# Two MLPs behind an attention, one core: another order on ScalarE and VectorE in the second unit of the second layer's later pairs

## The reference

```python
x = attn_out.reshape(B * S, D)                       # 6016 x 256
# first MLP
h = x @ w_in;  g = h * (1.0 / (1.0 + np.exp(-1.702 * h)));  x = g @ w_out
# second MLP
h = x @ w_in
g = np.where(h > 0.0, h, alpha * (np.exp(np.minimum(h, 0.0)) - 1.0))   # alpha = 1
return (g @ w_out).astype(np.float32)
```

## Time and profile before

| | us |
|---|---|
| median of 3 runs | 1035.35 |
| lowest and highest run | 1034.66, 1036.51 |
| the profiled execution, its own time | 1033.88 |
| its span in the profile | 1032.1 |
| PE busy in the span | 1023.7 |
| DVE busy | 762.9 |
| ACT busy | 760.8 |

### The profile page before, as it was taken

How to read it: one execution, slowest core, us unless ns; L and a number is a source line. 1 busy time by engine, 2 the same in 40 slices (tenths; PEclk the granted TensorE clock), 3 DMA queues, 4 the chain that set the end, 5 groups by cost and what they waited for, 6 DMA issues and landing times.

```text
span 1032.1 us, 14040 instructions
## 1 busy us (share of the span) xinstructions
PE 1023.7 (99%) x4636; PEld 860.1 (83%) x4636; DVE 762.9 (74%) x1244; ACT 760.8 (74%) x1362; POOL 26.1 (3%) x27
## 2 busy tenths in 40 slices
PE   8999999999999999999999999999999999999998
PEld 7878888888888888889998888888888888888996
DVE  6797766656656565655888988888888788788776
ACT  6996765565666566556688888788788788788885
POOL 3700000000000000000000000000000000000000
PEclk9999999999999999999999999999999999999999
DMA  8912012003003002003112002102102001110111
GB/s 328 325 38 55 1 41 42 0 21 62 1 1 80 1 1 59 1 1 122 42 61 98 1 1 62 21 1 62 21 1 62 15 6 38 20 21 1 21 22 36
DMA packets 103192, 46.25 MB, mean 45 GB/s; under 512 B 87184, under 2 KB 93776, under 8 KB 102480
## 3 DMA queue, kind: packets, MB, share of 16 engines
q1 hardware_dynamic: 102208, 44.12, 15.6%
q10 hardware_dynamic: 912, 1.25, 0.3%
HBM read 33.03 MB, written 12.32 MB: 44 GB/s over the span
## 4 chain that ended last, share of the span: by engine, by line
PE 98%; DMA 1%; ACT 0%; DVE 0%; SPq 0%; POOL 0%; issue 0%; ACTq 0%; DVEq 0%
PE bank L1155 32%; PE bank L1156 31%; PE bank L1157 31%; PE bank L1165 2%; DMA qk<-in_k_dram 1%; PE bank L1262 0%; PE bank L1263 0%; PE bank L1267 0%; SPq L337 0%; POOL qk_lo L441 0%; PE bank L1407 0%; ACT stage L470 0%; PE bank L1240 0%; PE bank L1178 0%; PE bank L1227 0%
## 5 line engine op out<-in xcount | busy, mean ns | idle before, releaser
L1155 PE MATMUL bank<-g_hi,w_dn_hi 128*128 128x512 f32 (+1 forms) x768 | 296.0, 385 | 0.0
L1156 PE MATMUL bank<-g_lo,w_dn_hi 128*128 128x512 f32 (+1 forms) x768 | 295.8, 385 | 0.0
L1157 PE MATMUL bank<-g_hi,w_dn_lo 128*128 128x512 f32 (+1 forms) x768 | 295.7, 385 | 0.0
L934 DVE TENSOR_TENSOR g_lo<-gated,g_hi 128x512 fp32r<-128x512 f32 (+1 forms) x384 | 259.8, 677 | 44.8 <-ACT g_hi L631 38.7
L1155 PE MATMUL bank<-blk_hi,w_up_hi 128*128 128x512 f32 (+1 forms) x672 | 260.2, 387 | 0.1
L1156 PE MATMUL bank<-blk_lo,w_up_hi 128*128 128x512 f32 (+1 forms) x672 | 258.9, 385 | 0.0
L1157 PE MATMUL bank<-blk_hi,w_up_lo 128*128 128x512 f32 (+1 forms) x672 | 258.8, 385 | 0.0
L631 ACT CAST g_hi<-gated 128x512 fp32r<-128x512 f32 (+1 forms) x288 | 175.8, 611 | 21.4 <-DVE gated L921 21.4
L1155 PEld LDWEIGHTS bank<-g_hi,w_dn_hi 128*128 128x128 f32 x768 | 144.2, 188 | 27.5 <-DVE g_lo L934 0.6
L1157 PEld LDWEIGHTS bank<-g_hi,w_dn_lo 128*128 128x128 f32 x768 | 144.2, 188 | 27.0
L1156 PEld LDWEIGHTS bank<-g_lo,w_dn_hi 128*128 128x128 f32 x768 | 144.2, 188 | 26.8
(11 more groups left out here) (125 smaller groups left out, 756.1 us busy)
## 6 DMA issues: line engine op xcount, KB each, us to landing
x_scratch<-xo SPq DMA_DIRECT2D x10, 512.0 KB, 3.1
raw<-x_scratch SPq DMA_DIRECT2D x5, 1024.0 KB, 4.9
out_dram<-blocks SPq DMA_DIRECT2D x40, 128.0 KB, 2.7
qk<-in_q_dram SPq DMA_DIRECT2D x13, 384.0 KB, 8.0
qk<-in_k_dram SPq DMA_DIRECT2D x12, 384.0 KB, 9.6
stage<-in_moe_w_in_dram SPq DMA_DIRECT2D x8, 512.0 KB, 7.7
stage<-in_moe_w_out_dram SPq DMA_DIRECT2D x8, 512.0 KB, 4.8
blocks<-in_v_dram SPq DMA_DIRECT2D x32, 128.0 KB, 3.3
```

What stands on the lines that cost most here:

```text
L934: nc.vector.tensor_tensor(g[1][:, x, 0:w], gated[:, n % 2, 0:w], g[0][:, x, 0:w].bitcast(F32), ALU.subtract).then_inc(c_glo, 1)
L1155: nc.tensor.matmul(out_ps, w_hi, x_hi, start=start, stop=False, skip_group_check=goes_on)
L1156: nc.tensor.matmul(out_ps, w_hi, x_lo, start=False, stop=False, skip_group_check=goes_on)
L1157: return nc.tensor.matmul(out_ps, w_lo, x_hi, start=False, stop=stop, skip_group_check=goes_on)
```

## The change

For the units with s > 6 and u = 1 (U = 57, 65, 73, 81, 89) ACT and DVE get an order of their own. ACT: copy_u1(U), Relu and Exp (U-1, H12), evacuate(s-1, 1), copy_u2(U), g_hi (U-1, H21), Relu and Exp (U, H11), copy_u3(U), g_hi (U, H11), and from there as before. DVE: sum12_of(U-1), elu (U-1, H21), g_lo (U-1, H22), sum11_of(U), elu (U-1, H12), g_hi (U-1, H12), g_lo (U-1, H21), g_lo (U-1, H12), elu (U, H11), g_lo (U, H11), sum22_of(U), elu (U, H22). All other units, and PE's, SP's and POOL's lists, stay as they are. No instruction is added or dropped.

```diff
@@ scalar, unit(U) @@
-                if u == 1 and s >= 1:
+                if u == 1 and s > NP:
+                    nonlinear(U - 1, H12)
                     evacuate(s - 1, 1)
-                if U - 1 < LAYER:
+                    copy_u2(U)
                     g_hi(U - 1, H21)
-                    gelu(U - 1, H12)
+                    nonlinear(U, H11)
+                    copy_u3(U)
+                    g_hi(U, H11)
                 else:
...
@@ vector, unit(U) @@
-                g_lo(U - 1, H21)
-                if U > LAYER:
+                if U // UNITS > NP and U % UNITS == 1:
                     elu(U - 1, H12)
-                g_hi(U - 1, H12)
-                if LAYER < U < ALL:
+                    g_hi(U - 1, H12)
+                    g_lo(U - 1, H21)
+                    g_lo(U - 1, H12)
                     elu(U, H11)
-                g_lo(U - 1, H12)
+                else:
...
```

More of the change, by code:

```diff
@@ L758, in unit @@
                     copy_u1(U)
-                if u == 1 and s >= 1:
+                if u == 1 and s > NP:
+                    nonlinear(U - 1, H12)
                     evacuate(s - 1, 1)
-                if U - 1 < LAYER:
+                    copy_u2(U)
                     g_hi(U - 1, H21)
-                    gelu(U - 1, H12)
-                else:
[L765 to L777, removed]
+                    nonlinear(U, H11)
+                    copy_u3(U)
+                    g_hi(U, H11)
+                else:
+                    if u == 1 and s >= 1:
+                        evacuate(s - 1, 1)
+                    if U - 1 < LAYER:
+                        g_hi(U - 1, H21)
+                        gelu(U - 1, H12)
+                    else:
+                        elu_first(U - 1, H12)
+                        g_hi(U - 1, H21)
+                        elu_second(U - 1, H12)
+                    if U == ALL:
+                        return
+                    nonlinear(U, H11)
+                    copy_u2(U)
+                    g_hi(U, H11)
+                    if u == 0:
+                        block_hi(s, T4)
+                    if U == LAYER - 1:
+                        dn_hi(2 * FB - 2)
+                    copy_u3(U)
                 side(U)
@@ L1119, in unit @@
                     sum11_of(U)
-                g_lo(U - 1, H21)
-                if U > LAYER:
+                if U // UNITS > NP and U % UNITS == 1:
                     elu(U - 1, H12)
-                g_hi(U - 1, H12)
-                if LAYER < U < ALL:
+                    g_hi(U - 1, H12)
+                    g_lo(U - 1, H21)
+                    g_lo(U - 1, H12)
                     elu(U, H11)
-                g_lo(U - 1, H12)
+                else:
+                    g_lo(U - 1, H21)
+                    if U > LAYER:
+                        elu(U - 1, H12)
+                    g_hi(U - 1, H12)
+                    if LAYER < U < ALL:
+                        elu(U, H11)
+                    g_lo(U - 1, H12)
                 if U == ALL:
```

## The result

| | changed | before, same comparison | ratio, 95% interval |
|---|---|---|---|
| first comparison, 9 and 9 runs | 1032.74 us | 1034.66 us | 0.998 (0.9972 to 0.9988) |
| second, 11 and 32 runs | 1033.68 us | 1034.0 us | 0.9996 (0.9987 to 1.0005) |
| third, 11 and 33 runs | 1033.53 us | 1034.82 us | 0.9982 (0.9973 to 0.9991) |

In the first comparison, the one that the prediction was about, the changed kernel is 1.9 us faster, 0.20%, and the interval doesn't hold 1. The forecast was 1033.7 us, 0.16% faster, with "no difference" as the likeliest verdict. The profiled execution took 1032.74 us, its span is 1031.0.

A forecast was written before the change was run, and what follows sets the result against it. TensorE, busy 99% of the span, was taken to bound the kernel. 1.8 us removed less about 0.15 given back took the profiled 1033.88 to 1032.2; the median's 1.5 above that gave 1033.7 us, range 1032.6 to 1035.2.

The forecast's parts named there:

- What bounds, and the prize: TensorE, busy 99%; its starts lost to late product5 and product7 loads in five units: 4 x 0.34 + 0.44 = 1.8 us.
- Part 1: ACT's Relu and Exp of (U-1, H12) ahead of the evacuation: product5's load no longer waits, 0.8 us to spare.
- Part 2: Evacuation behind that Exp: down H22's load 0.03 us late, last pair 0.13; costs 0 to 0.1, last 0.03 to 0.15.
- Part 3: copy u2 behind the evacuation, at product6's end: product7's load gets 1 us of room, down H21's 0.4 us.
- rival (c): product5 and product7 freed, but g_lo of H21 late for down H21: 1035.2 us; chance 0.09.
- Part 4: copy u3 ahead of g_hi (U, H11) delays sum22; next unit starts 0.55 us late on ACT, costing 0 to 0.1 per pair.
- Rival (a): Later sum22 makes next unit's copy u2 0.2 to 0.3 us late, product7 waits: 1034.3 us; chance 0.18.
- The price of lateness: At TensorE's weight loads, each may be about 0.1 us late at no cost; lateness beyond that is lost.
- The rule set beside the trace: Skill's 215.7 ns per 512-column matmul, against the trace's 0.2267 us: prize would be 2.1 us; the sum used the trace.
- net of 1.65 us: Whole kernel: 1.8 us removed, about 0.15 given back at the evacuation and in the next unit.
- the level: Median before, 1035.35 us, taken 1.5 above the profiled execution; the same difference added to 1032.2 gives 1033.7.
- (d): Matmul step really shorter, or lost starts pull more work forward: 2.1 to 2.3 us gained, 1033.1 us; chance 0.08.

The follow-up runs named there:

- the kernel with nothing late: Changed kernel with the evacuations back in front of Relu and Exp of (U-1, H12), and sum22 ahead of g_lo (U, H11): 1032.25 us, ratio 0.9982.
- the vector-only kernel: Changed kernel with ScalarE's order put back as before, only VectorE's new order kept in the five units: ratio 1.0009, run again 1.0003.

## Why the prediction came out as it did

- **What bounds, and the prize** (1.8 us): right. With nothing late in the later pairs the stretch is 1.88 shorter.
- **Part 1**: right in place and time; elu of H12 has 0.88 us of room, 0.8 was read.
- **Part 2, the evacuation**: right that this is the tightest place, and a little short. For a full pair 0.03 late was read and 0.05 came, which cost 0.02 to 0.03; for the last 0.13 was read and 0.15 came, which cost 0.06. The signal took about 0.08 us from the end of the evacuation's first half to the load in the last pair, where 0.05 was read from a copy, and the first 0.1 us of lateness was not quite free.
- **Part 3**: right; copy u2 starts at product6's end, g_lo of H21 was in time (its load was not late), so rival (c) didn't come.
- **Part 4, the delay handed on**: right in its path and size (0.58 us at the next copy u1, 0.55 read). It makes no load late in the full pairs, and product7's in the last by 0.13 us, at a cost of 0.03; "some 0.1 late, 0 to 0.05 lost" was read. Rival (a) didn't come. What is given back, 0.26 to 0.38 us against the kernel with nothing late, is above the 0.15 taken. In the first changed trace the late loads named here account for 0.2 of it: 0.11 in the full pairs' evacuations, 0.06 in the last one's, 0.03 in the unit behind.
- **The price of lateness**, lateness less 0.1, was drawn from two waits and holds from 0.3 to 1.1 us. Below that it isn't nothing: 0.05 late cost 0.02 to 0.03, and 0.15 cost 0.06.
- **The rule set beside the trace.** The Trainium skill's 215.7 ns a matmul, from "TensorE: Matmul & The Clock Gate", section "Wait — 56ns, not 53.3ns?", would have made the prize an estimated 2.1 us. The runs don't agree with it: the largest gain of any stretch is 1.88, and with no load late the step is still 0.2267 us. The trace's step was the right one to use.
- **Where it was wrong: the verdict.** The step that failed is "a measurement of this kernel can tell about 0.2% (2.1 us) from no change", for which the prediction gave no working. From it came "no difference" with 0.66 and "faster" with 0.27. Nine runs a side gave an interval of 0.08% to either side, which a gain of 0.16% clears, and the kernel was faster beyond it (0.998, 0.9972 to 0.9988). A net of 1.65 us should have been forecast as faster by 0.1 to 0.2%, a small gain and not none. How sure that would have been is another matter: of the three comparisons of the changed kernel one, 0.9996, takes in 1, and 1.9 and 0.3 us by medians lie on either side of the 1.5 to 1.6 that each trace holds.
- **A term of the sum that was off: the level.** The median before was put 1.5 us above the profiled execution, from three runs. Nine runs put it at 1034.66, 0.8 above. That makes 0.7 of the 1.0 us by which 1032.74 lies under the forecast's 1033.7; the other 0.3 is the first comparison's 1.9 against the net 1.65, more than its own trace holds (1.62). So 1032.74 lies only just inside the range. The mechanism and the net are right all the same, and a slip in the chances (half of (d)'s 0.08 taken as 0.05) changes nothing.

Left open: why a 448-column unit takes one of two lengths, and what brought the medians of the second comparison to within 0.3 us of each other. The start and the second length are each large enough for it, but only one of the eleven executions has a trace, so their share is argued, not shown. Open too is how the gain beyond copy u2's divides among g_hi, elu and copy u3.

## What to carry to other kernels

On an engine that is 99% busy, look at the waits of its loads and convert them to starts lost: here 3.2 us of waiting was 1.8 us of time, since 0.04 us stands before every load anyway and each of the ten late ones had about 0.1 us of slack. Before moving a drain of an accumulator behind other work, try the plain order first: putting the blocked copy and the last nonlinearity next to what they wait for gave all of the gain, and the evacuation in front was safer and 0.2 to 0.3 us better. Judge a change of a tenth of a per cent by a stretch of the trace that holds only the change, and work out what the measurement can tell from the runs that it will have, before "no difference" is forecast.

## What the runs showed of the hardware that I had not expected

The step of a 448-column matmul has two lengths, 0.2027 us (unit of 9.12 for 45 matmuls) and 0.2067 us (9.30), with the granted clock at 1.00 in both stretches, no load waiting, and the same instructions. In the first layer's last pair the longer one began in the middle of the pair in seven of the fourteen profiles, which made the time from the first copy u1 to that of U = 56 0.6 us longer (561.4 against 560.8). In the second layer's last pair it stood in two, once in the kernel before and once in the vector-only kernel. It isn't tied to the order of ACT and DVE. In the first layer it may go with the chip: of the twelve traces whose chip is on record, none of the four on one chip has it, three of the four on the second, and all four on the third. In the second layer it came in one of four on each of the latter two. The undisturbed units of 512 columns took 10.20 us in every trace, 45 steps of 0.2267.
